# One mLSTM-and-MoE kernel: q times d on VectorE, a third v buffer, batch 0's x moved inside SBUF

## The reference

```python
for t in range(S):                       # S = 768, per (b, h); D = 40
    m_new = maximum(f[t] + m, i[t])
    f_stab, i_stab, m = exp(f[t] + m - m_new), exp(i[t] - m_new), m_new
    C = f_stab * C + i_stab * outer(v[t], k[t])
    n = f_stab * n + i_stab * k[t]
    h = C @ q[t]
    y[t] = sigmoid(o[t]) * h / maximum(abs(n @ q[t]), 1)
x = y as [1536, 320]
x = softplus(x @ w_in) @ w_out           # 320 -> 2048 -> 320
e = argmax(x @ w_gate)                   # top-1 of 8 experts
out = gate_w * eom * (relu(x @ w1[e]) @ w2[e])
```

## Time and profile before

| | us |
|---|---|
| median of 3 runs | 419.03 (419.0 to 421.14) |
| profiled execution | 417.85 |
| its span | 416.1 |
| TensorE busy | 386.2 (93%) |
| VectorE busy | 283.7 (68%) |
| ScalarE busy | 225.9 (54%) |
| GpSimd busy | 212.2 (51%) |

### The profile page before, as it was taken

One profiled execution on the slowest core, in us unless ns is written; L12 is line 12 of the kernel. 1 busy time (PEld: TensorE's weight loads), 2 busy tenths in 40 slices (PEclk: granted clock), 3 DMA queues, 4 the chain that ended last, 5 costly groups with the idle time before them and its releaser, 6 DMA issues.

```text
span 416.1 us, 9463 instructions
## 1 busy us (share of the span) xinstructions
PE 386.2 (93%) x2741; PEld 359.5 (86%) x2742; DVE 283.7 (68%) x496; ACT 225.9 (54%) x406; POOL 212.2 (51%) x225
## 2 busy tenths in 40 slices
PE   0999996899999999999999999599999999999983
PEld 0858886789999999999999999588998999899873
DVE  8999989958656788557766676677473257874231
ACT  4647772454556545655555655546465358874230
POOL 6577978436556665342434464045264423886221
PEclk9999997899999999999999999989999999999998
DMA  7979774335255544644222254225736219741110
GB/s 198 304 286 320 231 221 147 112 83 165 76 182 172 184 134 153 189 135 166 72 71 61 66 202 143 105 64 174 277 117 260 64 40 354 262 153 36 56 36 26
DMA packets 30682, 63.43 MB, mean 152 GB/s; under 512 B 8984, under 2 KB 20763, under 8 KB 30012
## 3 DMA queue, kind: packets, MB, share of 16 engines
q1 hardware_dynamic: 28780, 57.61, 42.6%
q0 software_dynamic: 1808, 5.31, 3.8%
q10 hardware_dynamic: 64, 0.15, 0.1%
HBM read 56.40 MB, written 6.88 MB: 152 GB/s over the span
## 4 chain that ended last, share of the span: by engine, by line
PE 83%; DVE 8%; issue 2%; DMA 2%; ACT 2%; DVEq 0%; POOL 0%; SPq 0%; POOLq 0%; ACTq 0%
PE ps L1541 7%; PE ps L1543 7%; PE ps L1542 7%; PE ps L1525 5%; PE ps L1527 5%; PE ps L1526 5%; PE ps L1674 4%; PE ps L1676 4%; PE ps L1675 4%; PE ps L1631 3%; PE ps L1633 3%; PE ps L1632 3%; PE ps L1658 3%; PE ps L1532 3%; PE ps L1533 3%
## 5 line engine op out<-in xcount | busy, mean ns | idle before, releaser
L1156 DVE SCALAR_TENSOR_TENSOR gsum<-ps,soft 128x384 f32<-128x384 f32 x64 | 35.7, 557 | 51.8 <-ACT soft L897 51.5
L670 POOL TENSOR_TENSOR win_lo<-win_raw,win_hi 128x256 fp32r<-128x256 f32 x32 | 25.1, 783 | 85.6 <-DVE win_hi L1143 85.6
L889 ACT ACTIVATE soft<-ps 128x384 f32<-128x384 f32 x64 | 31.5, 492 | 68.5 <-PE ps L1533 68.4
L1541 PE MATMUL ps<-wout_hi,ghi 128*128 128x336 f32 x192 | 61.1, 318 | 1.0 <-DVE glo L1162 1.0
L1542 PE MATMUL ps<-wout_lo,ghi 128*128 128x336 f32 x192 | 60.7, 316 | 0.0
L1543 PE MATMUL ps<-wout_hi,glo 128*128 128x336 f32 x192 | 60.7, 316 | 0.0
L1525 PE MATMUL ps<-xhi,win_hi 128*128 128x384 f32 x128 | 43.6, 341 | 0.8 <-DVE gsum L1156 0.8
L1527 PE MATMUL ps<-xhi,win_lo 128*128 128x384 f32 x128 | 43.3, 338 | 0.0
L1526 PE MATMUL ps<-xlo,win_hi 128*128 128x384 f32 x128 | 43.2, 338 | 0.0
L1674 PE MATMUL ps<-split,hthi 128*128 x120 | 38.3, 319 | 1.9 <-DVE htlo L1333 1.9
L737 POOL DMA_INDIRECT out<-yout,token x15 | 17.7, 1177 | 41.3 <-DVE yout L1341 40.3
(11 more groups left out here) (214 smaller groups left out, 996.2 us busy)
## 6 DMA issues: line engine op xcount, KB each, us to landing
e1raw<-w_e SPq DMA_DIRECT2D x24, 512.0 KB
e2raw<-w_e SPq DMA_DIRECT2D x16, 640.0 KB, 5.2
win_raw<-w_in SPq DMA_DIRECT2D x32, 192.0 KB, 2.6
wout_raw<-w_out SPq DMA_DIRECT2D x32, 160.0 KB, 2.1
kq<-kq_t SPq DMA_DIRECT2D x16, 240.0 KB
wout_t<-w_out_t SPq DMA_DIRECT2D x3, 1024.0 KB, 14.1
og<-o_t SPq DMA_DIRECT2D x2, 1152.0 KB, 7.4
kr<-k_rows SPq DMA_DIRECT2D x8, 240.0 KB, 4.7
```

The source lines that it names most:

```text
L1156: dve.scalar_tensor_tensor(half(gsum, hf), ps[:, hf, 0:S // 2], 0.0, half(soft, hf), ALU.max, ALU.add).then_inc(g_done, 1)
L1541: pe.matmul(o, ghi[u][:, cols], wout_hi[u][:, :], start=False, stop=False, skip_group_check=True)
```

## The change

- *q times d.* `queries` moves from GpSimd to VectorE: for pair 0 after the scans of pair 1, for pair j+1 directly ahead of weigh(j+1), for pair 7 ahead of weigh(7) behind the first normalising. GpSimd waits for it (`wait_queries`) ahead of keys(j+1).
- *v1* gets a third buffer. inputs(j) and gate_column(j) wait for the outputs of pair j-3 instead of j-2.
- *Stores.* Of batch 0, SP moves the outputs of each pair straight from `stage` to `xn` (2, 3, 2 and 5 DMAs for the four pairs) and of both batches the sums straight to `den` (two DMAs a pair, one per head). `load_early`, `load_late` and the load of batch 1's `den` are gone. Batch 1's outputs go through DRAM as before.
- *Normaliser.* Its first store stands ahead of load_rows(7) and store_pair(3), its second ahead of store_pair(4). The spreads of tile 0 get a semaphore of their own. Batch 1's 12 spreads are split by x tile into three groups of 4, between the tile loads 3, 4 and 5.
- *Gates.* VectorE multiplies tiles 0 and 2 of batch 0's x by the gate, GpSimd tile 1. All low parts come after all normalising.
- *First tile.* ScalarE casts the first `win_hi` after its iteration 4, and GpSimd splits it in its round 5. `first_hidden` runs all products with `xhi` first, tile by tile and for both halves, and then those with `xlo`.
- *Start.* VectorE zeroes one q buffer, ScalarE the other two from a column of zeros, and GpSimd `f_start`.
- GpSimd's loop over tiles 4 to 6 is unrolled, and some SBUF places move.

The core of the diff:

```diff
@@ vector
+            def queries(j):
+                u = j % 2
+                dve.wait_ge(kq_loaded[j % 3], 32 * (j // 3) + 32)
+                dve.wait_ge(cast_read, D_CAST[j])
+                if j >= 2:
+                    dve.wait_ge(pv_done, j - 1)
+                dve.tensor_tensor(qd[u][:, :], kq[j % 3][:, 1, :], d_all[u][:, :], ALU.mult).then_inc(qd_done, 1)
...
+            queries(0)
             for j in range(PAIRS - 2):
                 states(j)
                 for h in range(2):
                     scan(j + 2, h)
                 if j == 4:
-                    normaliser(0, slice(0, 16 * EARLY), nq_early, 16, 0)
+                    normaliser(0, slice(0, 16 * EARLY), (1, 2), 0)
                 if j == 5:
-                    normaliser(0, slice(16 * EARLY, P), nq_loaded, 16, 1)
+                    normaliser(0, slice(16 * EARLY, P), (3,), 1)
+                queries(j + 1)
                 weigh(j + 1)
...
             states(PAIRS - 2)
-            high_in(0, 0, 16)
-            first_gate()
+            open_tile(0)
+            open_tile(2)
             normalise(0)
+            queries(PAIRS - 1)
             weigh(PAIRS - 1)
             states(PAIRS - 1)
             normalise(1)
-            low_part(0)
             normalise(2)
-            low_part(1)
-            low_part(2)
+            for k in range(KT):
+                low_part(k)
@@ gpsimd
             for j in range(1, PAIRS - 1):
-                queries(j)
+                wait_queries(pool, j)
                 keys(j + 1)
                 inputs(j + 1)
+                if j == 5:
+                    split_in(0, 0)
+                    pool.wait_ge(win_split, 2)
+            wait_queries(pool, PAIRS - 1)
             output_gate(0, 1)
-            queries(PAIRS - 1)
-            output_gate(0, 2)
@@ sync
             def store_pair(j):
                 sp.wait_ge(num_done, j + 1)
                 for h in range(2):
+                    at = 16 * (2 * j + h - H * b)
+                    sp.dma_start(den[at:at + 16, b, :], stage[u][HALF * h + D:HALF * h + V1, :].rearrange("o (p n) -> o p n", n=NQ)).then_inc(den_stored[u], 16)
+                for h in range(2):
+                    if b == 0:
+                        for k, at, first, n in head_pieces(2 * j + h):
+                            rows = slice(HALF * h + first, HALF * h + first + n)
+                            sp.dma_start(xn[at:at + n, k, :], stage[u][rows, :]).then_inc(stage_stored[u], 16)
+                    else:
+                        sp.dma_start(attn_rows[(2 * j + h - H) * D:(2 * j + h - H + 1) * D, :], stage[u][HALF * h:HALF * h + D, :]).then_inc(stage_stored[u], 16)
...
             store_pair(2)
             load_rows(6)
-            load_early()
             load_kq(7)
+            store_normaliser(0, 0, EARLY, 1, rden_early)
+            load_rows(7)
             store_pair(3)
-            load_rows(7)
-            store_normaliser(0, 0, EARLY, 1, rden_early)
-            load_late()
             sp.wait_ge(rden_early, 16)
-            spread_normaliser(0, 0, EARLY, rb_early)
+            for piece in spreads(0, EARLY):
+                spread(0, piece, rb_first if piece[0] == 0 else rb_early)
+            store_normaliser(0, EARLY, H, 2, rden_stored)
             store_pair(4)
-            store_normaliser(0, EARLY, H, 2, rden_stored)
             sp.wait_ge(rden_stored, 16)
-            spread_normaliser(0, EARLY, H, rb_loaded)
+            for piece in spreads(EARLY, H):
+                spread(0, piece, rb_loaded)
@@ tensor
+            def first_hidden():
+                pe.wait_ge(win_split, 2)
+                pe.wait_ge(p_done, 2 * PAIRS)
+                for k in range(KT):
+                    pe.wait_ge(xhi_done, k + 1)
+                    for hf in range(2):
+                        pe.matmul(o, hi[:, k, :], xhi[0][:, k, half(hf)], ...)
+                        if k < 2:
+                            pe.matmul(o, lo[:, k, :], xhi[0][:, k, half(hf)], ...)
+                for hf in range(2):
+                    for k in range(KT):
+                        if hf == 0:
+                            pe.wait_ge(xlo_done, k + 1)
+                        last = pe.matmul(o, hi[:, k, :], xlo[0][:, k, half(hf)], ...)
+                    last.then_inc(h_ready, 1)
```

246 lines of the change are left out of this document (137 added, 109 removed).

## The result

| | before | after |
|---|---|---|
| median in the same comparison, us | 422.06 (20 runs, 418.41 to 427.62) | 417.62 (20 runs, 416.09 to 420.19) |
| profiled execution, us | 417.85 | 417.35 |
| its span, us | 416.1 | 415.5 |
| start of the second hidden tile, us | 85.63 | 83.56 |
| weighing of pair 4, 5, 6, 7 starts, us | 48.55, 58.23, 66.94, 75.06 | 50.55, 58.46, 66.25, 71.93 |

What follows compares the result with a forecast made beforehand. VectorE was taken as the bound from 48.5 to 81.79 us, half its excess being time shared with GpSimd. Low parts 3.8 us earlier and 0.3 to 0.4 from the softplus gave 4.2 us off 419.03: 414.8 us, range 413.2 to 417.8.

Steps and rivals of the forecast that it cites:

- the price of SP's queue: SP in the attention stage: more issues per pair at some 0.33 us each, seven loads fewer; no wait taken.
- everything later should move as a block: After the second hidden tile starts at 85.6 us, the rest of the kernel only shifts with it.
- q times d on VectorE: Attention pairs: eight products of 0.92 us added to VectorE, eight of 1.82 to 2.92 us taken from GpSimd.
- The pace of pairs 1 to 4: Attention pairs 1 to 4: VectorE's period becomes 6.57 us, beside TensorE's 6.53.
- Third v buffer: GpSimd's inputs in the attention stage: zero by itself, but the condition for q times d at 0.92 us.
- rival (c): GpSimd still busy when queries come: four of seven products cost 1.6 us more, so slower, 421.2 us; chance 0.07.
- Moves inside SBUF: Normaliser's sums and x skip DRAM: VectorE's 0.99 us wait goes; 1.3 us kept in the range for late sums.
- The tail: VectorE from pair 4's weighing to the last low part: that part ends at 77.96 us, 3.8 us earlier.
- Rival (a): TensorE's clock still falls before pair 7's scores: 2.1 us of the gain remain, 416.9 us; chance 0.12.
- Rival (b): A transfer takes over: spreads for heads 6 and 7, or pair 3's sums, 1.5 us late, 416.3 us; chance 0.12.
- The cover in the first MoE product: Reordered spreads and GpSimd's unrolled loop lie under busy TensorE: zero, at worst some 0.5 us.
- The sum: At the second hidden tile: 4.2 us earlier than 85.63, giving 414.8 us for the kernel; chance 0.62.

Runs made afterwards that it cites:

- after_again: The changed kernel unaltered, timed and profiled a second time: median 418.04 us, ratio 0.9929 to the kernel before.
- rows: The changed kernel with the rows loads of pairs 4 to 6 issued ahead of the stores of pairs 0 to 2: 417.71 us, ratio 0.9917.
- rows_pool: The kernel of rows with q times d back on GpSimd: 421.38 us, ratio 1.0011 to the kernel before.
- qd_pool: The changed kernel with q times d back on GpSimd: 420.38 us, ratio 0.9964 to the kernel before.
- v2: The changed kernel with two v buffers instead of three: 420.22 us, ratio 0.9964 to the kernel before.
- qd_v3: The kernel before with only q times d on VectorE and a third v buffer: 421.04 us, ratio 1.0007.
- warm: The changed kernel with 12 products of zeros on TensorE ahead of pair 7's d cast: 417.40 us, ratio 0.9907 to the kernel before.
- parts: The changed kernel with the second part of the first expert's weights issued ahead of tile loads 5: 418.24 us, ratio 0.9924 to the kernel before.
- qd_alone: The kernel before with only q times d moved to VectorE, two v buffers kept: 420.01 us, ratio 0.9986.

## Why the prediction was right or wrong

*The step that failed* is the price of SP's queue. The text had "some 0.33 us each" for the issues of the moves, took no wait behind them, and let the second store of the normaliser leave at 64.4 and the rows land in time. An issue took 0.6 to 1.0 us. The second store left at 67.41, and VectorE waited for its spreads by 1.00 and 0.43 us; pair 5's rows came 1.0 us late in after, and pair 4's 2.2 us late in after_again, this last for a reason that SP's order does not remove (see rows). VectorE's last low part was laid out to end at 77.96 and ended at 79.67 and 79.71, 1.7 us late in both profiles. In after 1.0 of it is the wait for the spreads, and the rest came from the start and the pace of pairs 1 to 4; in after_again 1.8 is the step from pair 4 to pair 5 and 0.4 the spreads, less what was gained elsewhere. The second step that failed is "everything later should move as a block": from the second hidden tile on the kernel took 1.5 and 3.1 us more than before.

| us | laid out | after | after_again |
|---|---|---|---|
| weighing of pair 4 starts | 49.45 | 50.55 | 49.16 |
| weighing of pair 5 starts | 57.38 | 58.46 | 58.85 |
| weighing of pair 7 starts | 71.22 | 71.93 | 72.54 |
| last low part ends | 77.96 | 79.67 | 79.71 |
| second hidden tile starts | 81.43 | 83.56 | 82.84 |
| from there to the end of the span | 330.5, as before | 331.9 | 333.6 |

*q times d on VectorE.* Right in its durations: 0.89 to 0.96 us where GpSimd was idle, scans of two at 3.38 us, weighings at 1.82 whatever GpSimd did. Right in sign: 3.7 us by rows and rows_pool, whose intervals are apart, and 1.5 to 2.3 us by qd_pool, whose interval overlaps that of after_again. The Trainium skill (GPSIMD Engine Reference, section 1, Specifications) names VectorE's instructions with two SBUF inputs, or in a 2-port performance mode, as those that contend. The traces agree for two inputs (a gate product at 2.56 us for 0.92), and the PSUM-fed weighing stays at 1.82. The normaliser's first operation has one tensor input and took 1.65 for 0.15 us in rows_pool; no trace here tells which mode it ran in.

*The pace of pairs 1 to 4.* Forecast 6.57 us. In after_again the steps to pairs 2, 3 and 4 are 6.37, 6.36 and 6.95, in after 6.92, 6.79 and 6.53. Right, where nothing came late; the steps of after are 0.17 us longer on average than 6.57.

*Third v buffer.* The step that said "zero by itself" was wrong as a price. Without it about half of the gain goes (v2), as the inputs wait and fall beside the scans. The text had it as a condition, and rival (c) described what happens without it.

*Moves inside SBUF.* The wait for the sums went in after (0.99 to none); it was back where the rows were loaded ahead of the stores (0.43 us in rows, 1.45 in rows_pool), and a move of the sums lands 2.8 us after its issue in the median of after. Wrong was "some 0.33 us each" for the issue: pairs 0 to 3 cost SP 2.9, 4.2, 2.8 and 5.4 us for 4, 5, 4 and 7 issues. Their price came where the text had not looked, at the rows of pair 5, which held GpSimd for 1.0 us, so that its inputs ran beside the scans and these took 0.8 us longer (4.15 for 3.38), and at the spreads. The 1.8 us of after_again (9.69 for 7.93) hang on the rows of pair 4; the first reading, that SP's stores made these late as well, was refuted by rows. The Trainium skill (DMA: Bandwidth & Descriptors, Issuing engines are not separate DMA queues) calls the time to initiate a DMA usually small relative to the DMA. Here one issue takes 0.7 to 0.95 us of a DMA that lands 2.8 us after it, a quarter to a third, and the five issues of pair 1 hold SP for 4.2 us.

*What the moves were worth* was too low in the text, not too high: in qd_v3, where the sums still go through DRAM, the 2.3 us gained at pair 7's weighing are given back to the spreads.

*The tail.* From pair 5 on VectorE ran as laid out: 7.79 and 5.68 us for 7.93 and 5.91. It came 1.1 us later than laid out, as pair 4 already did (50.55 for 49.45). Half of that is the start (below): pair 1 was weighed at 30.31 where 28.87 and the 0.9 us of the queries give 29.8. The other half is the three steps at 6.75 us instead of 6.57. From pair 4 to 5 it took 7.91 us, as the longer scans were paid for by the normaliser, 0.80 us (56.85 to 57.65) for the 1.36 reckoned.

*Rival (a)* came true in after and not in after_again, where the stop ahead of the same scores was 0.64 us and the clock stayed at 1.00. In after TensorE stood still for 1.09 us, not 3.28, and the clock fell for some 4 us all the same. Scores, updates and outputs took 5.3 us instead of 3.8 (2.26, 1.13 and 1.93 for 1.61, 0.73 and 1.48). Of these 1.5 us some 0.8 reached the end of the stage (3.89 for 3.13 us, see warm).

*Rival (b)* came true in part: the normaliser's second store left at 67.41 instead of 64.4 and the spreads of heads 6 and 7 at 70.86, because the issues ahead of them cost double, and VectorE waited 1.00 us. It cost nothing at the end of the stage in after, as TensorE was late itself: it ran without a stop from the outputs of pair 7 (75.68) through all products of high parts to those of low parts. In qd_v3, where the same wait is 1.73 us, TensorE did stop. Rivals (a) and (b) hid each other in after, so each has to be priced in a kernel where the other is gone.

*The cover in the first MoE product.* "Zero, at worst 0.5 us" was wrong: 1.3 us in after and 1.0 in after_again, behind a win tile that landed late. Part of it may be the weight part that went from one side of `tile_loads(0, 5)` to the other, which could be read in the diff; but kernels with the part moved back lost 0.5 to 1.4 us at the same place, so the cause is open.

*The start.* In after, TensorE waited 1.81 and 1.31 us for wout_t and then ran at half clock. That isn't shown to be the change's: after_again, parts, rows and v2 ran 14 to 28 us at 1.00, and qd_alone and qd_v3, with before's start, didn't. It costs up to 0.8 us at pair 1 (30.31 against 29.48 in after_again).

*The routing stage* followed none of the text's terms. From its first product to the first product of the experts it took 12.0 us in before, 11.7 in after and 13.6 in after_again, and its clock (262 to 285 us) was 0.93, 0.93 and 0.78. The longer form, 13.5 to 14.1 us at 0.78, is there in six of the eight profiles of kernels that have the whole change, and in none of the other six. So it may belong to the change, by the moment at which the stage is reached; no run tested it. It takes back 1.6 us in after_again, and single profiles of one kernel differ by as much as the terms looked for.

*The sum.* 4.2 us were forecast at the second hidden tile; 2.1 us (after) and 2.8 us (after_again) are seen in the profiles. Of the missing 2.1 us in after 1.7 are VectorE's lateness and 0.4 the clock's fall; in after_again 1.7 are lateness, of which 0.3 came back as the second hidden tile followed the low parts sooner than laid out. Then the rest of the kernel took more time than before, and the whole spans are 415.5 and 416.4 us against 416.1: the profiles show 0.6 us gained and 0.3 us lost, while the ratio shows 3.4 us gained. The rest isn't in the profiles compared. It fits that the profiled execution of before was shorter than any of its timed runs: in its other runs GpSimd's products must cost more, as the spread of qd_pool (9.3 us against 3.0) suggests. That is argued and not shown, as only one profile of before was taken. So that the forecast of 4.2 us came near the measured gain is luck in part: a term that was too large met one that was left out. The absolute 414.8 us is 2.8 us under the measured median for a second reason as well, its base of three runs, 419.03, against 422.06.

## What to carry to other kernels

Before work is moved to an engine that has no slack, look at what else must be there first: here q times d on VectorE gained nothing alone (0.9986) and nothing with the third buffer (1.0007), while all parts together gave 0.8%, and about half of that without the third buffer (0.9964). Count what a queue pays to issue a DMA, by the kind of DMA, and look at every load that stands behind it; then test whether the order is what makes a load late, as here one left 3.8 us earlier and released its reader only 0.5 us earlier. Compare whole spans as well as the stretch that was changed. Where GpSimd and VectorE share their time, compare medians of many runs, since one profile shows only one of the ways in which their instructions can meet.

## What the runs showed of the hardware

- Issuing a move from SBUF to SBUF held SP for 0.7 to 0.95 us a piece in the lines shown of after (1.89 for 2, 2.15 for 3, 4.19 for 5), a load or spread from DRAM for 0.36 to 0.53, a store of the normaliser for 0.32. The move of the sums landed 2.8 us after its issue in the median.
- A load of 240 KB left at 34.96 and released its reader at 44.07 (rows), with the DMA engines 94% busy; one of the same rows left at 38.78 and released it at 44.59 (after_again).
- TensorE's granted clock fell from 2.4 to 1.2 GHz after it had stood still for only 1.09 us (after, 67.1 to 68.2 us) and stayed there for some 4 us. It fell after 1.26 us in after_again (50.19), and did not fall after stops of 0.99 and 1.18 us in after (75.68, 83.56).
- A VectorE operation with one SBUF tensor input and 48 columns took 1.65 us beside GpSimd (rows_pool) and 0.15 without (after). It ended at 57.99 and GpSimd's product at 57.94; in before the same operation ended at 57.32 and the product at 57.27. So what costs looks like the wait for GpSimd's instruction, not the operation's own length.
- GpSimd is slowed as well: the same keys took 1.02 us beside the weighing and 3.83 beside the scans.
